# Row-tiled pairs in place of full matmuls: two FFN products interleaved on TensorE

## What is computed

```python
w = softmax(weight_gen, axis=-1)                    # (2, 4096, 8, 7)
x = sum over k of w[..., k] * x_pad[s + k]          # (8192, 192)
h = x @ w_in;  x = (h * cos(h)) @ w_out             # 192 -> 2048 -> 192
h = x @ w2_in; out = maximum(0.01 * h, h) @ w2_out  # 192 -> 2048 -> 192
```

## Time and profile before

| | |
|---|---|
| median of 3 runs | 1267.12 us (1266.32 to 1267.42) |
| profiled execution, its own time | 1268.98 us |
| span of its profile | 1267.0 us |
| TensorE (PE) busy | 1230.7 us, 97% |
| VectorE (DVE) busy | 1074.0 us, 85% |
| ScalarE (ACT) busy | 842.4 us, 66% |
| GpSimd (POOL) busy | 97.3 us, 8% |
| mean granted TensorE clock | 0.988 |

### The profile page before, as it was taken

How to read it: one execution, slowest core, us unless ns; L and a number is a source line. 1 busy time by engine, 2 the same in 40 slices (tenths; PEclk the granted TensorE clock), 3 DMA queues, 4 the chain that set the end, 5 groups by cost and what they waited for, 6 DMA issues and landing times.

```text
span 1267.0 us, 15397 instructions
## 1 busy us (share of the span) xinstructions
PE 1230.7 (97%) x5464; PEld 1005.2 (79%) x5464; DVE 1074.0 (85%) x973; ACT 842.4 (66%) x911; POOL 97.3 (8%) x50
## 2 busy tenths in 40 slices
PE   7789889999999999999999999999999999999998
PEld 4667668888888888888888888888888888888886
DVE  7898999979797997979799797988979798897854
ACT  1668558486675857668495766849576685857753
POOL 4865320000000000000000000000000000000000
PEclk9799999999999999999999999999999999999999
DMA  9021000100001010010101001010100101000000
GB/s 218 34 76 56 1 32 1 44 1 13 31 0 43 0 43 0 0 43 0 43 0 43 0 0 43 0 43 0 43 0 0 43 0 43 0 12 1 1 13 25
DMA packets 10581, 31.47 MB, mean 25 GB/s; under 512 B 836, under 2 KB 5314, under 8 KB 10304
## 3 DMA queue, kind: packets, MB, share of 16 engines
q1 hardware_dynamic: 10560, 31.19, 7.8%
HBM read 24.89 MB, written 6.29 MB: 25 GB/s over the span
## 4 chain that ended last, share of the span: by engine, by line
PE 85%; DVE 11%; issue 1%; ACT 1%; DMA 1%; SPq 0%; ACTq 0%; DVEq 0%
PE acc_b L880 8%; PE slot L854 8%; PE acc_b L881 8%; PE acc_a L871 8%; PE acc_a L873 8%; PE acc_a L872 8%; PE slot L855 8%; PE slot L856 8%; PE slot L858 8%; PE slot L857 8%; DVE g_lo L662 3%; DVE gate L734 2%; DVE prods L290 2%; DVE prods L296 1%; DVE gate L742 1%
## 5 line engine op out<-in xcount | busy, mean ns | idle before, releaser
L509 ACT ACTIVATE g_hi<-gate 128x1024 fp32r<-128x1024 f32 x256 | 271.4, 1060 | 161.9 <-PE acc_a L873 66.3
L662 DVE TENSOR_TENSOR g_lo<-gate,g_hi 128x1024 fp32r<-128x1024 f32 x256 | 329.7, 1288 | 16.3 <-ACT g_hi L509 16.2
L880 PE MATMUL acc_b<-g_hi,out_hi_lo 128*128 128x512 f32 x512 | 204.5, 399 | 14.4 <-DVE g_lo L662 12.0
L734 DVE SCALAR_TENSOR_TENSOR gate<-gate,turns 128x1024 f32<-128x1024 f32 x128 | 165.1, 1290 | 59.8 <-ACT gate L586 59.0
L558 ACT ACTIVATE turns<-slot 128x1024 f32<-128x1024 f32 x128 | 131.1, 1024 | 122.5 <-PE slot L858 122.5
L751 DVE TENSOR_TENSOR gate<-slot,gate 128x1024 f32<-128x1024 f32 x128 | 156.6, 1223 | 64.0 <-ACT gate L608 63.5
L854 PE MATMUL slot<-x_a_hi,in_a_lo 128*128 128x512 f32 x512 | 202.6, 396 | 6.1 <-DVE gate L751 6.0
L871 PE MATMUL acc_a<-g_hi,out_hi_lo 128*128 128x512 f32 x512 | 200.6, 392 | 2.5 <-DVE g_lo L662 2.5
L881 PE MATMUL acc_b<-g_lo,out_hi_lo 128*128 128x512 f32 x512 | 201.4, 393 | 0.0
L873 PE MATMUL acc_a<-g_hi,out_hi_lo 128*128 128x512 f32 x512 | 200.4, 391 | 0.0
L872 PE MATMUL acc_a<-g_lo,out_hi_lo 128*128 128x512 f32 x512 | 200.2, 391 | 0.0
(11 more groups left out here) (76 smaller groups left out, 1279.3 us busy)
## 6 DMA issues: line engine op xcount, KB each, us to landing
x_win<-in_x SPq DMA_DIRECT2D x14, 960.0 KB
out<-result SPq DMA_DIRECT2D x16, 384.0 KB, 2.3
raw_out<-in_moe_w_out SPq DMA_DIRECT2D x1, 1536.0 KB, 20.2
raw<-in_moe_w_out SPq DMA_DIRECT2D x4, 384.0 KB, 3.3
raw_in_a<-in_moe_w_in SPq DMA_DIRECT2D x1, 1024.0 KB, 13.9
raw_in_b<-in_moe_w_in SPq DMA_DIRECT2D x2, 512.0 KB, 16.1
raw<-in_moe_w_in SPq DMA_DIRECT2D x2, 512.0 KB, 5.0
raw<-in_moe_w_in SPq DMA_DIRECT2D x4, 256.0 KB, 3.9
```

What stands on the lines that cost most here:

```text
L509: nc.scalar.activation(g_hi[:, q % 2, :], gate[:, q % 2, :], ACT.Copy)\
L662: nc.vector.tensor_tensor(g_lo[:, q % 2, :], gate[:, q % 2, :], g_hi[:, q % 2, :].bitcast(FP32), ALU.subtract)\
L880: nc.tensor.matmul(acc_b[:, :], both, hi, start=f == 0, stop=False)
```

## The change

Every product runs as pairs of matmuls on 64 rows, one on partitions 0 to 63 and one on 64 to 127, each into another PSUM bank. A pair stands for one full matmul. The two halves of a 128-row term go to the same bank at different times. The lowest term of rows b (64 rows) is a half-height matmul for each of the two tiles and the two make one pair; for this `in_b_lo` is packed to half its columns and rows b's high part is copied a second time to partitions 64 to 127 (`x1_up`, `x2_up`). So a unit's two products are 19 pairs. One procedure interleaves the first product of unit q with the second of unit r = q - 3, with `slot[:, 0]`, `slot[:, 1]`, `acc_a`, `acc_b` as P0, P1, A, B:

```diff
+            def both_products(i, q, j, r, wait_for_next=None):
...
+                wait_to_fill(i, q)
+                for k in range(4):
+                    half_product(0, P0, *first[0][k], start=k == 0)
+                    half_product(1, P1, *first[1][k], start=k == 0)
+                half_product(0, P0, b_lo, x_b)
+                half_product(1, P1, b_lo, x_up).then_inc(tiles_done, 1)
+
+                wait_to_sum(i, r, before)
...
+                    pe.wait_ge(summed, unit(i, r, before))
+                for k in range(4):
+                    half_product(0, B, *b[k], start=v == 0 and k == 0)
+                    ins = half_product(1, A, *a[k], start=v == 0 and k == 0)
+                ins.then_inc(tiles_done, 1)
+                pe.wait_ge(tiles_done, done + 1)
+                for k in range(2):
+                    half_product(0, P1, *first[1][k])
+                    ins = half_product(1, A, *a[4 + k])
+                ins.then_inc(tiles_done, 1)
+                if v == len(FIRST_UNITS) - 1:
+                    pe.wait_ge(tiles_done, done + 2)
+                    for k in range(2):
+                        half_product(0, P1, *first[1][2 + k], stop=k == 1)
+                        half_product(1, B, *b[k])
+                    pe.wait_ge(tiles_done, done + 3)
+                    for k in range(2):
+                        half_product(0, A, *a[k])
+                        ins = half_product(1, B, *b[2 + k], stop=k == 1)
+                    ins.then_inc(summed_b, 1)
+                    for k in range(4):
+                        sum_a = half_product(0, A, *a[2 + k], stop=k == 3)
+                        fill_p = half_product(1, P0, *first[0][k], stop=k == 3)
+                    sum_a.then_inc(summed, 1)
+                    fill_p.then_inc(filled, 1)
                 else:
+                    for k in range(2):
+                        half_product(0, P1, *first[1][2 + k], stop=k == 1)
+                        half_product(1, P0, *first[0][k])
+                    pe.wait_ge(tiles_done, done + 3)
+                    for k in range(2):
+                        half_product(0, A, *a[k])
+                        ins = half_product(1, P0, *first[0][2 + k], stop=k == 1)
+                    ins.then_inc(filled, 1)
+                    if wait_for_next is not None:
+                        wait_for_next()
+                    for k in range(4):
+                        half_product(0, A, *a[2 + k])
+                        ins = half_product(1, B, *b[k])
+                    ins.then_inc(summed, 1)
```

```diff
+            def rest_of_iteration(i, q):
+                after = UNITS[q] + 1
+                if after == OUTPUT_STEP and kind(i, after) == "output":
+                    both_products(i, q, i, q - LAG, lambda: wait_for_output(i))
+                    transpose_output(slots[OUTPUT_STEP % SLOTS])
+                elif after == INPUT_STEP and kind(i, after) == "input":
+                    both_products(i, q, i, q - LAG, lambda: wait_for_input(i, INPUT_STEP))
+                    transpose_input(slots[INPUT_STEP % SLOTS])
+                else:
+                    both_products(i, q, i, q - LAG)
```

The transposes are done on 64 rows each too: 16 in place of 8 for the input, 12 in place of 6 for the output, in pairs. On ScalarE the copies to `x1_up` and `x2_up` are added, T(s+1) moves behind S(s), and the output's and input's copies move to the head of their step:

```diff
+                if kind(i, step) == "output":
+                    move_result(i, step, i - 2)
+                if step == INPUT_STEP and input_splits(i, step):
+                    act.wait_ge(filled, fills(i, step))
+                    split_high(i, step, i + 1)
                 in_first = kind(i, step) == "first"
...
                     act.wait_ge(summed, unit(j, 7) + 1)
...
-                first_read(i, step)
...
+                    leave_mid_a()
                 if in_first:
                     act.wait_ge(fraction, i * 8 + q + 1)
...
+                first_read(i, step)
+                if step == SECOND_OUT - 1 and (not isinstance(i, int) or i >= 2):
+                    act.wait_ge(summed, unit(i, 15, 1) + 1)
+                    leave_res_a()
```

More of the change, by code:

```diff
@@ L516, in pending_high, with split_high, leave_mid_a, leave_res_a @@
                     high_part(q, unit(i, q, b))
-            def split_high(i, step):
+            def split_high(i, step, chunk):
                 slot = slots[step % SLOTS]
[L521 to L526, removed]
+                a, b = slot[:, :, 0:N // 2], slot[0:DB, :, N // 2:N]
+                nc.scalar.activation(halves(x1_a_hi[:, :]), a, ACT.Copy).then_inc(x1_hi, 1)
+                nc.scalar.activation(halves(x1_b[0:DB, :]), b, ACT.Copy).then_inc(x1_hi, 1)
+                act.wait_ge(x1_hi, chunk * 3 + 2)
+                nc.scalar.activation(x1_up[DB:P, :], x1_b[0:DB, :].bitcast(FP32), ACT.Copy).then_inc(x1_hi, 1)
+            def leave_mid_a():
+                nc.scalar.activation(mid_a[:, :], acc_a[:, :], ACT.Copy).then_inc(acc_a_out, 1)
+            def leave_res_a():
+                nc.scalar.activation(
+                    res_a[:, :].rearrange("p (j k r) -> p k j r", j=J, k=2),
+                    acc_a[:, :].rearrange("p (k j r) -> p k j r", j=J, k=2), ACT.Copy)\
+                    .then_inc(acc_a_out, 1)
             def move_result(i, step, c):
@@ L570, in split_second_high @@
                         .then_inc(x2_hi, 1)
+                    nc.scalar.activation(x2_up[DB:P, :], mid_b[:, :], ACT.Copy)\
+                        .then_inc(x2_hi, 1)
             def step_of(i, step):
@@ L720, in step_of @@
                 here = kind(i, step)
+                if step == INPUT_STEP and input_splits(i, step):
+                    split_low(i, step, i + 1)
                 if is_unit(i, step):
@@ L883, in rows_b @@
                     return ins
[L886 to L892, removed]
-                else:
[L894 to L897, removed]
+                b = rows_b()
@@ new lines, in second_product, with pairs @@
+                if u == len(FIRST_UNITS) - 1:
+                    b.then_inc(summed_b, 1)
+                rows_a().then_inc(summed, 1)
+            def pairs(i, q):
+                if isinstance(i, int) and i == 0:
+                    return q - LAG
+                if isinstance(i, int) and i == 1 and q < LAG:
+                    return 8 - LAG + q
+                if isinstance(i, int) and i == LAST and q > 8:
+                    return i * 16 - 12 + q - 10
+                if isinstance(i, int) and i == LAST:
+                    return i * 16 - 12
+                return i * 16 - (12 - q)
@@ new lines, in wait_to_fill, with wait_to_sum @@
+                if q == 8:
+                    pe.wait_ge(x2_ready, i * 2)
+                    pe.wait_ge(x2_hi, i * 3)
+                    if isinstance(i, int) and i == 1:
+                        pe.wait_ge(w2_lo, sum(LOS[:IN_PIECES]))
+            def wait_to_sum(i, q, before=0):
+                pe.wait_ge(lo_ready, unit(i, q, before) + 1)
+                n = i - before if isinstance(i, int) else HEAD
+                if n == 0 and q == 0:
+                    pe.wait_ge(w1_out_lo, 8)
+                if n == 1 and q == 8:
+                    pe.wait_ge(w2_lo, sum(LOS))
+                if q in (0, 8) and n > 0:
+                    phase = first_phase(i, before) if q == 0 else second_phase(i, before)
+                    pe.wait_ge(acc_a_out, phase)
+                    pe.wait_ge(acc_b_out, phase)
@@ new lines, in operands, with fill_alone, sum_alone, wait_for_input @@
+            def operands(q):
+                if q < 8:
+                    return W1, x1_a_hi, x1_a_lo, x1_b, x1_up
+                return W2, x2_a_hi, x2_a_lo, x2_b, x2_up
+            def fill_alone(i, q):
+                wait_to_fill(i, q)
+                first_product(*operands(q), q % 8, slots[UNITS[q] % SLOTS])
+            def sum_alone(i, q, before=0):
+                wait_to_sum(i, q, before)
+                second_product(W1 if q < 8 else W2, q % 8, q % 2)
+            def wait_for_input(i, step):
+                wait_for_slot(i, step)
+                pe.wait_ge(att, i * ATT_STEPS + 2 * ATT_STEPS)
@@ L963, in keep_clock, with iteration @@
+            def iteration(i):
+                for q in range(LAG):
+                    both_products(i, q, i - 1, q - LAG + len(UNITS))
+                for q in range(LAG, len(UNITS)):
+                    rest_of_iteration(i, q)
             def keep_clock(n):
```

290 lines of the change are left out of this document (145 added, 145 removed).

## The result

The kernel after takes **1283.5 us** (median of 4 runs, 1282.39 to 1285.18), the one before 1266.72 in the same comparison: ratio 1.0133, 95% interval [1.0115, 1.0151]. The forecast was 1283.

What follows compares the result with a forecast made beforehand. TensorE's own stream was taken as the loop's bound; pairs, transposes, three waits and restarts gave 75.50 us per iteration against 74.38, +15.7 us over 14 iterations on 1267.1, rounded to 1283 us. The range was 1246 to 1302 us.

Steps and rivals of the forecast that it cites:

- Pairs: TensorE's loop stream: a pair costs as much as a full matmul, taken as 0.230 us; 304 pairs are 69.92 us per iteration.
- Transposes: Input and output transposes in each iteration, as pairs with the same number of weight columns: 1.54 us as before.
- `tiles_done`: TensorE's waits for itself in the loop: nothing, with up to 1.3 us per iteration for the upper end.
- (A): TensorE waits for ScalarE to empty `acc_a` into `mid_a` after unit 7: 1.54 us per iteration.
- (B): TensorE waits for ScalarE to empty `acc_a` into `res_a` after unit 15: 0.59 us per iteration.
- (C): The attention on VectorE ends too late for the input transposes, so TensorE stands 1.65 us per iteration.
- Short restarts: Short restarts of TensorE in the loop: 0.26 us per iteration, left over from the kernel before.
- Sum of the loop: Pairs, transposes, three waits and restarts: 75.50 us per iteration against 74.38, +1.12, or +15.7 us over 14 iterations.
- My own low end: The forecast's own case at a pair spacing of 0.2268 us: waits 4.01 us, iteration 74.76 us, time 1272 us.
- The start and the end: First 190 us: nothing, or 3 us either way; there and in the last iteration, gain and waits cancel.
- that the gain comes through: Rival: TensorE's loop waits stay under 2.66 us per iteration and the kernel gets faster, 1260 or 1230 us; chance 0.28.
- TensorE's issue: Rival: four instructions per pair make instruction issue the loop's bound, +2.0 us per iteration, 1311 us; chance 0.06.

Runs made afterwards that it cites:

- e4: Against the kernel after: e2's ScalarE order, plus the attention's instructions handed out earlier, two more before unit 7 ends; 1243.49 us, ratio 0.9814 to the kernel before.
- e6: e4 with the `add_pairs` moved from step 9 to 8 and iteration 1's softmax sum of row group 2 ahead of L(14); 1240.57 us, ratio 0.9788.
- e2: Against the kernel after: ScalarE empties `acc_a` first at both hand-overs, ahead of its other reads; 1270.88 us, ratio 1.0034 to the kernel before.
- e3: Against the kernel after: the edits of e1 and e2 together; 1272.14 us, ratio 1.0040 to the kernel before.
- e1: Against the kernel after: one `add_pairs` of the attention moved from step 11 to step 10; 1268.62 us, ratio 1.0008 to the kernel before.
- e7: Against the kernel after: the two products not interleaved, each unit 18 full matmuls and one pair; 1330.29 us, ratio 1.0500 to the kernel before.

## Why the prediction was right, point by point

- **What bounds before**: TensorE's stream: it was busy 966.92 of 967.00 us. In e4 and e6 the iteration comes within 2.2 and 2.0 us of pairs and transposes alone (69.9).
- **Pairs**: that a pair costs as much as a full matmul was right. The term was mis-sized: I took 0.230, the long stream has 0.2267, its lower end. That is 304 x 0.0033 = 1.0 us per iteration, 14 us in all, too much.
- **Transposes**: "1.54 us as before"; they cost 0.44 for the output and 0.53 for the input, 0.97, 0.6 less. The term went by the columns of the weights and left out those that stream through: 64 per transpose in place of 128 (64x64 above, 128x128 in the earlier trace rows).
- **`tiles_done`**: nothing, as said. The timeline shows no gap at these waits in the stretch above.
- **(A), (B), (C)**: all three came, at the places and with the releasers forecast; e2 shows that ScalarE's order is the cause of (A) and (B), and e4 that the attention's place is that of (C). Idle 1.5, 0.5 and 1.8 us by the profile's waits. Counted as I did, from spacing to spacing, they are 534.49 - 532.62 less 0.23 = 1.64; 0.65 as above; 552.28 - 550.11 less 0.23 = 1.94: 4.23 us, against 3.78 forecast at 0.230 and 4.01 at 0.2268. The chains were right to 0.2 us; a faster stream makes its waits longer, so an error in the spacing is in part given back.
- **Short restarts**: 0.26 was left for them; 74.88 - 304 x 0.2267 - 0.97 - 4.23 leaves 0.8. Behind each stand and behind the transposes the next pairs come slower than the stream, 0.12 us over 11 pairs behind (A).
- **Sum of the loop**: 68.92 + 0.97 + 4.23 + 0.76 = 74.88 and not 75.50, +0.43 per iteration and not +1.12. The 13 iterations from M(0) of iteration 2 to that of 15 took 975.8 us against 969.4: +6.4, of which 1.5 is one fall of the clock; the first of them is 0.2 shorter than before. The forecast had 15.7 for 14. My own low end (74.76 us, 1272) was near for the loop.
- **The start and the end**: here a step failed. "There and in the last iteration the pairs' gain and a last (A) and (B) cancel" and "nothing, or 3 us either way": the start lost 5.4 us, and from M(0) of iteration 15 to the end are 114.6 us against 112.0, 2.6 more. The waits of PE in that last stretch are 3.6 us against 0.9, a last (A) and (B) (1.5 and 0.5) among them, and no gain of the pairs made them good. So in the profiles the loop adds 4.9, the start 5.4, the end 2.6 and the fall 1.5, in all 14.4 (forecast 15.7). By the medians it is 16.8, as the profiled execution before stands 2.3 above its median. The total was right because errors cancelled: a loop priced some 11 us too high, and 9.5 us outside its terms that were put at nothing. The sign was right by the three waits: without them the iteration would be some 4 us shorter.
- **Rivals**: that the gain comes through was wrong for this kernel; that it would take fewer waits was right (e4, e6). The prediction gave it 0.28 because 1.1 us in 3.78 turn the sign; the margin in the loop was in fact 0.43 us of 4.23. TensorE's issue was no bound: a pair is four instructions and its spacing is that of one matmul. Pairs do overlap.

## What to carry to other kernels

Before paying for a faster stream on the bounding engine, move each of its signals and waits to its new place and add up, from the start of the matmul that gives the signal, what the other engines have in order between it and the wait; here three sums of two to twelve terms told the sign. Buffers that are emptied between two phases (`acc_a`, `acc_b`) are to be emptied first, ahead of reads that have slack, and background work is to be begun where its engine idles. Then a change that lost 1.3% wins 2.1%. The kernel before had hardly anything to win by such moves in its loop, where TensorE was busy 966.92 of 967.00 us.

## What the runs showed of the hardware that was not expected

- Two half-height matmuls in different banks start up to 0.06 us apart (537.11 and 537.16) and still keep a spacing of 0.2267 us per pair over 15 pairs.
- A stand of TensorE of 1.9 us was in 11 of 13 iterations of e3 followed by some microseconds at the lower level of its clock (granted clock 0.62 and 0.82 in the 3 us stretches behind it), which cost another 1.6 us, nearly as much as the stand. In e2's profile 2 of 13 stands of 2.0 us were followed so; after stands of 1.0 us (e1) no iteration of the profile was longer than the rest. The Trainium skill, "TensorE: Matmul & The Clock Gate", HAM oscillation, warns that idle gaps between bursts of matmuls can bring the clock down. The trace agrees that they do; the gaps in the page's example are longer than these, so by this case shorter ones can do it too.
- Going from full to half height and back costs 0.40 us (e7). The Trainium skill, "TensorEngine Tiling (Array Packing)", Key Properties, says that changing the tiling mode drains TensorE; the trace agrees in that the change costs time, and gives the price.
